# Reordering the opening and the passage to the experts, and stacking k by plane, in an attention, routing and two-layer kernel

## The reference

```python
q_rot, k_rot = rotate(q), rotate(k)                    # cos/sin tables
attn = softmax(q_rot @ k_rot.T / sqrt(64))             # per batch and head
x = (attn @ v) laid out as 2304 rows of 512
logits = (x / |x|) @ (emb / |emb|).T / tau             # 8 experts
expert = argmax(logits); gate = softmax(logits)[expert]
y = gate * (relu(x @ w1[expert]) @ w2[expert])
h = y @ w_in
out = (h - tanh(h)) @ w_out
```

## Time and profile before

| | us |
|---|---|
| median of 3 runs | 1074.96 |
| lowest, highest | 1074.87, 1075.3 |
| the profiled execution | 1075.3 |
| its span in the profile | 1073.5 |
| TensorE busy | 985.6 |

### The profile page before, as it was taken

How to read it: one execution, slowest core, us unless ns; L and a number is a source line. 1 busy time by engine, 2 the same in 40 slices (tenths; PEclk the granted TensorE clock), 3 DMA queues, 4 the chain that set the end, 5 groups by cost and what they waited for, 6 DMA issues and landing times. The chain is left out here.

```text
span 1073.5 us, 18569 instructions
## 1 busy us (share of the span) xinstructions
PE 985.6 (92%) x5624; PEld 874.8 (81%) x5625; DVE 597.3 (56%) x1196; ACT 582.1 (54%) x1276; POOL 424.6 (40%) x228
## 2 busy tenths in 40 slices
PE   2799999999998399999999949999999999999996
PEld 2799899899997378888888838889989898898985
DVE  5577777777776751111111116776666666666664
ACT  2577777777776542232222226665665666655553
POOL 2998878888710249569957041000000000000000
PEclk9899999999999599999999979999999999999999
DMA  8767656566732455324431043210000000000001
GB/s 238 188 192 195 176 156 168 168 184 168 254 109 70 155 211 177 118 82 148 143 110 60 21 150 98 64 43 30 1 29 0 0 29 0 29 0 0 30 1 30
DMA packets 57202, 107.99 MB, mean 101 GB/s; under 512 B 18240, under 2 KB 23872, under 8 KB 54848
## 3 DMA queue, kind: packets, MB, share of 16 engines
q1 hardware_dynamic: 49552, 89.61, 28.3%
q0 software_dynamic: 3440, 11.27, 3.5%
q10 hardware_dynamic: 4160, 6.44, 1.7%
HBM read 61.89 MB, written 17.03 MB: 74 GB/s over the span
## 5 line engine op out<-in xcount | busy, mean ns | idle before, releaser
L1620 PE MATMUL hd_ps<-y_hi,w_hi 128*128 128x384 f32 x384 | 131.7, 343 | 8.2 <-DVE g_sb L1789 8.2
L1689 ACT ACTIVATE mag<-hd_ps 128x384 f32<-128x384 f32 x96 | 47.2, 492 | 152.8 <-PE hd_ps L1620 150.4
L1620 PE MATMUL hd_ps<-y_lo,w_hi 128*128 128x384 f32 x384 | 129.9, 338 | 0.0
L1620 PE MATMUL hd_ps<-y_hi,w_lo 128*128 128x384 f32 x384 | 129.9, 338 | 0.0
L990 DVE TENSOR_REDUCE neg_max<-ps 128x1 f32<-128x576 f32 x144 | 108.0, 750 | 30.0 <-PE ps L573 27.4
L1006 DVE TENSOR_TENSOR pt_lo<-ps,pt_hi 128x512 fp32r<-128x512 f32 x144 | 99.2, 689 | 44.4 <-ACT pt_hi L765 42.8
L765 ACT ACTIVATE pt_hi<-ps 128x512 fp32r<-128x512 f32 x144 | 86.8, 604 | 61.1 <-PE ps L620 59.7
L1638 PE MATMUL o_ps<-w_hi,g_hi 128*128 128x512 f32 x288 | 114.9, 399 | 2.2 <-DVE g_lo L1798 2.2
L1798 DVE TENSOR_TENSOR g_lo<-g_sb,g_hi 128x384 fp32r<-128x384 f32 x96 | 53.5, 558 | 112.9 <-ACT g_hi L1704 112.9
L1638 PE MATMUL o_ps<-w_lo,g_hi 128*128 128x512 f32 x288 | 114.4, 397 | 0.0
L573 PE MATMUL ps<-k_st,q_st 128*128 128x288 f32 x512 | 94.3, 309 | 21.7 <-DMA q_st<-qk_split 19.5
(11 more groups left out here) (220 smaller groups left out, 2346.6 us busy)
## 6 DMA issues: line engine op xcount, KB each, us to landing
k_st<-qk_split SPq DMA_DIRECT2D x64, 288.0 KB, 4.6
raw_qk<-in_qk SPq DMA_DIRECT2D x14, 1152.0 KB, 5.3
w_stage<-in_w SPq DMA_DIRECT2D x28, 512.0 KB, 3.5
q_st<-qk_split SPq DMA_DIRECT2D x60, 144.0 KB, 3.4
y_rows<-y_row ACTq DMA_DIRECT2D x20, 256.0 KB, 2.1
raw_v<-in_v SPq DMA_DIRECT2D x32, 128.0 KB, 2.3
w_stage<-in_w_in SPq DMA_DIRECT2D x8, 512.0 KB, 3.5
token_rows<-in_w_out SPq DMA_DIRECT2D x16, 256.0 KB, 2.7
```

The costliest lines, as they stand in the source:

```text
L1620: op = nc.tensor.matmul(hd_ps[f % 2][:, 0:G], w[:, c, cols], y[:, c, :], start=c == 0 and h == 0, stop=c == DC - 1 and h == 2)
L1689: nc.scalar.activation(mag[r][:], hd_ps[r][:, 0:G], ACT.Abs).then_inc(mag_done, 1)
```

## The change

- `k_st` (both planes of k in one buffer) becomes `k_hh` and `k_ll`; the k stacking is eight DMAs of 144 KB for a pair instead of four of 288 KB. With the four of q a pair has twelve, and `STACKS` follows. `hi` and `lo` become two buffers; addresses stay.
- In the opening the embeddings are loaded behind the tables; DVE squares them between the rotations of k and q; the root comes behind ScalarE's q stacking; the Newton steps stand behind the fifth maximum of pair 0; DVE scales `fold_sb` instead of GpSimd, ahead of its `body(0)`.
- The second half of the first expert's weights is issued in the attention block once all squares are done, instead of in the experts' block.
- GpSimd gathers tiles 1 to 12 at once, then, after the first set is split, tiles 13 to 20, and then splits the next set without gathers between.
- `tile_eq`, a temporary of the routing, lies elsewhere.

```diff
-AHEAD = 5
+AHEAD = HELD - 8
...
-        STACKS = 8 * 16
+        STACKS = 12 * 16
...
-        k_st = [[put(f"k_st{r}{u}", [P, 2, S], F32R) for u in range(2)] for r in range(2)]
-        k_hh, k_ll = ([[k_st[r][u][:, part, :] for u in range(2)] for r in range(2)] for part in range(2))
+        k_hh = [[put(f"k_hh{r}{u}", [P, S], F32R) for u in range(2)] for r in range(2)]
+        k_ll = [[put(f"k_ll{r}{u}", [P, S], F32R) for u in range(2)] for r in range(2)]
...
-        qk_split = put("qk_split", [P, 2, 2, S], F32R)
-        hi, lo = (qk_split[:, part, :, :] for part in range(2))
+        hi = put("qk_hi", [P, 2, S], F32R)
+        lo = put("qk_lo", [P, 2, S], F32R)
...
-        tile_eq = spots(nc, w_at + 3 * SET // 4)("tile_eq", [P, T, MT])
+        tile_eq = spots(nc, lo_at)("tile_eq", [P, T, MT])
...
             def stack_k(r, landed=None):
                 landed = landed or (stack_in[r], stack_in[r])
                 for u in range(2):
-                    both = qk_split[u * DH:(u + 1) * DH, :, 1, :].bitcast(F32)
+                    rows = slice(u * DH, (u + 1) * DH)
                     for half in range(2):
-                        sp.dma_start(k_st[r][u][half * DH:(half + 1) * DH, :, :].bitcast(F32), both).then_inc(landed[u], 16)
+                        to = slice(half * DH, (half + 1) * DH)
+                        sp.dma_start(k_hh[r][u][to, :].bitcast(F32),
+                                     hi[rows, 1, :].bitcast(F32)).then_inc(landed[u], 16)
+                        sp.dma_start(k_ll[r][u][to, :].bitcast(F32),
+                                     lo[rows, 1, :].bitcast(F32)).then_inc(landed[u], 16)
...
             sp.wait_ge(x_stored, 16 * 2 * (B + 1))
+            sp.wait_ge(sq_done, T)
+            for c in range(UP, CHUNKS):
+                sp.dma_start(early_half(rows, c), weight_chunk(a["w1"], a["w2"], expert, c)).then_inc(second_half[c - UP], 16)
...
             add_up(1, 0, 1, first=True)
-
-            pool.wait_ge(consts_in, 16 * 6)
-            pool.wait_ge(emb_scale, 1)
-            by_emb = emb_n[:, 4, :].unsqueeze(1).to_broadcast([P, PB, E])
-            nc.gpsimd.tensor_tensor(fold_sb[:, :, 0:E], fold_sb[:, :, 0:E], by_emb, ALU.mult)
-            nc.gpsimd.tensor_tensor(fold_sb[:, :, FW:FP], fold_sb[:, :, FW:FP], by_emb, ALU.mult).then_inc(fold_scaled, 1)
             split_v(0, 0, first=True)
...
-            act.dma_start(emb_sb[:], a["emb_t"].rearrange("(c p) e -> p c e", p=P)).then_inc(emb_in, 16)
             act.dma_start(cos_sb[:, 1, :], a["cos"]).then_inc(tables_in, 16)
             act.dma_start(sin_sb[:, 1, :], a["sin"]).then_inc(tables_in, 16)
+            act.dma_start(emb_sb[:], a["emb_t"].rearrange("(c p) e -> p c e", p=P)).then_inc(emb_in, 16)
             act.dma_start(tau_sb, a["tau"].partition_broadcast(P)).then_inc(tau_in, 16)
...
-            act.wait_ge(emb_clamped, 1)
-            nc.scalar.activation(emb_n[:, 1, :], emb_n[:, 0, :], ACT.Sqrt).then_inc(emb_root, 1)
-
             act.wait_ge(cleared, 1)
             act.wait_ge(rope_done, 1)
...
+            act.wait_ge(emb_clamped, 1)
+            nc.scalar.activation(emb_n[:, 1, :], emb_n[:, 0, :], ACT.Sqrt).then_inc(emb_root, 1)
...
+            dve.wait_ge(tables_in, 32)
+            rope_first(1, first_k_in, first_k_mult, first_k_done)
+
             dve.wait_ge(emb_in, 16)
             nc.vector.tensor_tensor(emb_sq[:], emb_sb[:], emb_sb[:], ALU.mult).then_inc(emb_squared, 1)
 
-            dve.wait_ge(tables_in, 32)
-            rope_first(1, first_k_in, first_k_mult, first_k_done)
+            dve.wait_ge(table_scaled, 2)
+            rope_first(0, first_q_in, mult_done, rope_done)
             dve.wait_ge(emb_summed, 1)
             nc.vector.tensor_scalar(emb_n[:, 0, :], norm_ps, 1e-30, None, ALU.max).then_inc(emb_clamped, 1)
-
-            dve.wait_ge(table_scaled, 2)
-            rope_first(0, first_q_in, mult_done, rope_done)
-
-            dve.wait_ge(tau_in, 16)
-            chain(nc.vector.reciprocal(inv_tau, tau_sb))
-            dve.wait_ge(emb_root, 1)
-            newton(chain, nc, emb_n[:, 2, :], emb_n[:, 1, :], emb_n[:, 0, :], emb_n[:, 3, :])
-            nc.vector.tensor_scalar(emb_n[:, 4, :], emb_n[:, 2, :], inv_tau, None, ALU.mult).then_inc(emb_scale, 1)
...
             for i in range(TILES):
                 maximum(0, 0, i)
+                if i == MIX:
+
+                    dve.wait_ge(tau_in, 16)
+                    chain(nc.vector.reciprocal(inv_tau, tau_sb))
+                    dve.wait_ge(emb_root, 1)
+                    newton(chain, nc, emb_n[:, 2, :], emb_n[:, 1, :], emb_n[:, 0, :], emb_n[:, 3, :])
+                    chain(nc.vector.tensor_scalar(emb_n[:, 4, :], emb_n[:, 2, :], inv_tau, None, ALU.mult))
+
+            dve.wait_ge(consts_in, 16 * 6)
+            by_emb = emb_n[:, 4, :].unsqueeze(1).to_broadcast([P, PB, E])
+            nc.vector.tensor_tensor(fold_sb[:, :, 0:E], fold_sb[:, :, 0:E], by_emb, ALU.mult)
+            nc.vector.tensor_tensor(fold_sb[:, :, FW:FP], fold_sb[:, :, FW:FP], by_emb, ALU.mult).then_inc(fold_scaled, 1)
             body(0, 0, first=True)
...
         @block.sync
         def _(sp):
-            expert = sp.value_load(plan[0:1, FIRST, 0:1], min_val=0, max_val=E - 1)
-            for c in range(UP, CHUNKS):
-                sp.dma_start(early_half(rows, c), weight_chunk(w1, w2, expert, c)).then_inc(second_half[c - UP], 16)
...
-            def two_more(c):
-                for t in range(AHEAD + 2 * c, min(AHEAD + 2 * c + 2, HELD)):
-                    gather(t)
...
-            with pool.If(last > 0):
-                slot = pool.value_load(plan[0:1, SLOT, 1:2], min_val=0, max_val=1)
-                split_set(0, slot, two_more)
-            with pool.If(last < 1):
-                for t in range(AHEAD, HELD):
-                    gather(t)
-            for t in range(AHEAD + 2 * CHUNKS, HELD):
+            for t in range(AHEAD, HELD):
                 gather(t)
-            with pool.Fori(1, 3) as before:
+            with pool.Fori(0, 3) as before:
                 next_set(before)
```

More of the change, by code:

```diff
@@ L146, in attention @@
         pt_lo = put("pt_lo", [P, FULL + 1, MAIN], F32R)
+        lo_at = w_at + 4 * (10 * S + 4 * WIDE + (FULL + 1) * WIDE_PT)
         v_split1 = put("v_split1", [P, TILES + 2, 2 * DH], F32R)
@@ L279, in attention @@
         emb_root = sem("emb_root")
-        emb_scale = sem("emb_scale")
         fold_scaled = sem("fold_scaled")
@@ L332, in stack_k @@
                 for u in range(2):
-                    both = qk_split[u * DH:(u + 1) * DH, :, 1, :].bitcast(F32)
+                    rows = slice(u * DH, (u + 1) * DH)
                     for half in range(2):
-                        sp.dma_start(k_st[r][u][half * DH:(half + 1) * DH, :, :].bitcast(F32), both).then_inc(landed[u], 16)
-            def stack_q(r):
[L338 to L341, removed]
+                        to = slice(half * DH, (half + 1) * DH)
[3 more added lines that the diff above has]
+                                     lo[rows, 1, :].bitcast(F32)).then_inc(landed[u], 16)
+            def stack_q(r):
+                for half, part in enumerate((hi, lo)):
+                    to = slice(half * DH, (half + 1) * DH)
+                    for u in range(2):
+                        sp.dma_start(q_st[r][u][to, u * TAIL:u * TAIL + S].bitcast(F32),
+                                     part[u * DH:(u + 1) * DH, 0, :].bitcast(F32)).then_inc(stack_in[r], 16)
             def store_tail(p, r):
@@ L830, in _ @@
             for u in range(2):
-                for half in range(2):
-                    act.dma_start(q_st[0][u][half * DH:(half + 1) * DH, u * TAIL:u * TAIL + S].bitcast(F32),
-                                  qk_split[u * DH:(u + 1) * DH, half, 0, :].bitcast(F32)).then_inc((first_a, stack_in[0])[u], 16)
+                for half, part in enumerate((hi, lo)):
+                    to = slice(half * DH, (half + 1) * DH)
+                    act.dma_start(q_st[0][u][to, u * TAIL:u * TAIL + S].bitcast(F32),
+                                  part[u * DH:(u + 1) * DH, 0, :].bitcast(F32)).then_inc((first_a, stack_in[0])[u], 16)
+            act.wait_ge(emb_clamped, 1)
+            nc.scalar.activation(emb_n[:, 1, :], emb_n[:, 0, :], ACT.Sqrt).then_inc(emb_root, 1)
             act.wait_ge(sums_set, 1)
@@ L1196, in _, with split_set @@
         def _(pool):
-            def split_set(before, slot, between=None):
+            def split_set(before, slot):
                 for c in range(CHUNKS):
-                    if between:
-                        between(c)
                     if c == 0:
```

## The result

The changed kernel takes 1083.52 us in the median of four executions (1081.81 to 1085.83), the kernel before 1074.91 beside it (1073.94 to 1075.3): a ratio of 1.0083, 95% interval 1.0062 to 1.0103, 8.6 us slower. The prediction said 1075.7 and a range of 1072.6 to 1079.0; it was wrong, on the side of too little loss.

The account below looks back on a forecast made before the run. The prediction took TensorE to bound the attention loop, so only shifted stage starts count: -0.75 (tables), +0.3 (k stacking) and +1.2 (first gather) sum to +0.75 us, 1075.7 on the median, range 1072.6 to 1079.

Parts of the forecast that it names:

- Newton steps and fold scaling moved: Opening, DVE: the moved small operations stay hidden by pair 1's stacking, value 0; without that cover up to 1.3 us.
- DVE's moved steps reaching body 0: Opening: listed sign that the prediction is wrong, the moved small operations delaying the first attention body; no size given.
- rival 1: Stacking of q and k: each small DMA costs its 0.98 us issue, delaying bodies; +9.1 us, 1084.1, chance 0.09.
- Tables ahead: Opening loads: cos and sin tables issued before the embeddings land earlier, gain 0.75 us (0.5 to 1.25).
- The price of that order: Opening, DVE: emb_sq between the two rotations might wait for the later emb_sb; value 0, bounds 0 and 1 us.
- k stacked by eight DMAs: Stacking of pair 1: more, smaller issues start body 0 later, +0.3 us (-1 to +4.1); in the loop 0.
- Early loads and the gather: Passage to the experts: first gather lands later beside the early weight loads, delaying the transposes 1.2 us (0 to 2.8).
- Gathers, second set, tile_eq: Experts, GpSimd: gathers issued together and set 1 split behind them make nothing wait, 0; tile_eq only moves.
- Clock: Body 0: a shorter stop ahead of it could keep the clock at 2.4 GHz, giving up to 2.8 us.
- rival 3: Opening and passage faster: earlier tables, shorter stacking, hidden gather, higher clock in body 0; 1072.0 us, chance 0.14.

Follow-up runs that it names:

- the combination with PSUM: Changed kernel with Newton steps in PSUM, emb_sq behind q's rotation, early loads back in the experts' block: ratios 0.9995, 1.0009; with k by four DMAs 0.9991, 0.9988.

## Why the prediction was wrong

**The step that failed** is "Newton steps and fold scaling moved": value 0, without cover up to 1.3, "no slower on DVE, I assume". I moved instructions with the durations they had at 16.3 to 17.57, when GpSimd was idle, to a place where GpSimd works without a break. Its first product in that profile:

```profile
20.34 2.68 POOL L507 TENSOR_TENSOR rotated<-by_cos,by_sin 128x1152 f32<-128x1152 f32 x1 [18.76 <-DVE by_sin L1070]
```

What the step measured: the seven small operations take 7.3 us in the first profile of the changed kernel, 8.5 in the second and 8.6 with the opening's edits alone, instead of 1.5, and 1.5 again with their operands in PSUM. Body 0 is 4.2, 6.6 and 7.1 us later by it, with the other edits of the opening. Terms and bounds knew of no such wait, and no rival held it; only the list of signs named its effect, DVE's moved steps reaching body 0. The number of rival 1, 1084.1, is close to the measured one by chance; its mechanism is refuted.

The trace of before had shown it. GpSimd and DVE in the experts' block, a tensor_scalar on 18 elements per partition, and the next operation, a reciprocal:

```profile
391.36 1.91 POOL L1212 TENSOR_TENSOR w_hi<-w_stage,one 128x1024 f32 x1
...
391.60 1.72 DVE L1484 TENSOR_SCALAR norm<-norm 128x18 f32<-128x18 f32 x1
...
393.35 0.27 DVE L1485 RECIPROCAL gate<-norm 128x18 f32<-128x18 f32 x1
```

L1484 ends at 393.32, when L1212 does at 393.27. The rule is also in the Trainium skill (SBUF — State Buffer, Who interferes with whom): DVE and GpSimd share a pair of SBUF ports, which one instruction holds to its end; a DVE operation with two inputs in SBUF, or one that can enter a two-port mode, as tensor_scalar can, contends with GpSimd for it, and one with at most one SBUF input outside those modes doesn't. The traces agree: L91 (two inputs) and L92 (tensor_scalar) were held up to 2.55 us, the reciprocals and the maxima from PSUM weren't, and L91 and L92 took 0.17 us once their inputs lay in PSUM.

**Tables ahead**: right in sign, 2.7 us where I had 0.75 (0.5 to 1.25); over all profiles DVE starts on the tables at 8.25 to 9.18 in the old order and at 6.06 to 6.43 in the new. **The price of that order**: `emb_sq` waited 3.73 and 2.27 us in the two profiles of the changed kernel, where my upper bound was 1. `emb_sb` was there at 13.57 and 12.18, not far from the 12 that I had taken, but DVE was done with k at 9.8 to 9.9 and not at 11.85: the larger gain made the larger wait. The q issue came at 17.43 and 16.05 (before 16.33), so the wait took all or nearly all of the gain. With it out of the way the q issue is 2.6 us earlier, of which 1.1 reach body 0.

**k stacked by eight DMAs**: +0.3 (-1 to +4.1), measured 0.0 from first issue to body 0 (10.11 against 10.10), and TensorE never waits for q_st or `k_ll` in the loop. The start of the twelfth issue was right (6.98 us after the first, I had 11 x 0.64 = 7.04); body 0 followed it by 3.1 us, where I took 3.4 for the landing.

**Early loads and the gather**: +1.2 (0 to 2.8), measured +1.9 in the changed kernel and +2.0 alone. The mechanism was right. The landing was 6.0 where I took 5.7, and the transposes don't follow it directly: the profile still names the sequencer, since the block ends some 0.4 us after the landing (368.71 + 6.0 = 374.7, GpSimd on at 375.06). The two make the 0.7 us that the term lacked. I had said it would name a DMA.

**Gathers, second set, tile_eq**: 0, measured 1.0001. **Clock** (in rival 3): in the first profile the granted clock stayed at 1.00, 2.4 GHz, through body 0, where it had been 0.84 on average, and the body took 18.88 us instead of 19.13. The up to 2.8 us that I gave to a higher clock weren't there. Over all fourteen profiles body 0 takes 18.4 to 19.1 us at 1.00 (nine of them) and 18.9 to 19.1 at 0.84 to 0.86 (five), so it takes about as long at either. What sets the length of a body wasn't looked for.

Sum of what was measured: +7.1 (opening) + 1.9 (passage) + 0 (planes) = +9.0, against +8.6 in the medians and +9.0 in the second profile. Whether the combination with PSUM is faster than the kernel before stays open: neither its times nor its profiles can tell.

## What to carry to other kernels

Don't move an operation with the duration that it had at its old place: look at what runs beside it at the new one, and between DVE and GpSimd ask of each small operation how many inputs it reads from SBUF and whether it is a tensor_scalar. Here the chain of small operations was kept free by putting its intermediate results in PSUM. A transfer that is started early is not free even if all that needs it is later: ask which short, urgent transfer (here a gather that the end of a whole block waits for once it lands late) it will run beside.

## What the hardware showed that I had not expected

- A DVE operation on 128x8 elements takes 0.17 us or up to 2.55 us, by where its operands are and what GpSimd does.
- The 16 KB of `emb_sb`, in pieces of 32 bytes, issued ahead of the two tables of 288 KB, held these up by 1.8 to 3.1 us (8.25 to 9.18 in five profiles against 6.06 to 6.43 in the nine of kernels that issue the tables first). Whether it is the small pieces wasn't tested.
- k stacked by four DMAs of 288 KB or by eight of 144 KB, with the same pieces: 10.0 to 10.2 us from SP's first issue to body 0 either way.
- In the passage the end of a block waits for a gather issued in it, though no instruction of that block does: with the early loads TensorE goes on 0.35 to 0.40 us after its landing.
- The dense stage takes some 6 us longer in four of the fourteen profiles (360.1 to 360.9 us against 352.9 to 354.5), of three kernels and the changed one among them; where it was looked at, the time goes at its start, in waits that the profile can't name. Its cause wasn't found.
